# Order of loads and rank items in a fused attention and two-layer kernel, with extra TensorE products at the start

## The reference

```python
a   = softmax(phi, axis=2)                       # phi: 8 x 8 x 576 x 32, over the 32 memory slots
k_m = einsum('bhsm,bhsd->bhmd', a, k)            # 32 x 64 per head
v_m = einsum('bhsm,bhsd->bhmd', a, v)
attn = softmax(q @ k_m^T / 8, axis=-1)           # 576 x 32 per head
x = (attn @ v_m), heads side by side             # 4608 x 512
h = x @ w_in;  g = where(h > 0, h, exp(min(h, 0)) - 1);  x = g @ w_out        # 512 -> 2048 -> 512
h = x @ w2_in; g = h * clip(h + 3, 0, 6) / 6;            out = g @ w2_out     # 512 -> 2048 -> 512
```

## Time and profile before

| what | value |
|---|---|
| median of three runs | 1538.38 us (1538.25 to 1538.83) |
| profiled execution, its time | 1538.7 us |
| profiled execution, its span | 1537.0 us |
| PE busy | 1499.0 us, 98% |
| DVE, ACT, POOL busy | 660.1, 623.5, 126.1 us |
| mean granted TensorE clock | 0.992 |
| L270 of the up passes (pT_hi, w_lo), x512 | 153.2 us busy, 14.4 us idle before |

### The profile page before, as it was taken

The page is one execution under the profiler, slowest core; times in us unless marked ns, Lnnn a source line. Parts: engine busy times, 40 slices in busy tenths (PEclk is TensorE's granted clock), DMA queues, the critical chain, the costliest instruction groups (busy, mean ns, idle before and its releaser), DMA issues.

```text
span 1537.0 us, 24660 instructions
## 1 busy us (share of the span) xinstructions
PE 1499.0 (98%) x9680; PEld 1306.2 (85%) x9680; DVE 660.1 (43%) x1180; ACT 623.5 (41%) x1284; POOL 126.1 (8%) x85
## 2 busy tenths in 40 slices
PE   3999999999999999999999999999999999999999
PEld 2889989889998989999988888888888888888887
DVE  4456565555656556555432222323232222323222
ACT  2655555555555555566632222222222222222222
POOL 0310000000000000003730000101010010101000
PEclk8899999999999999999999999999999999999999
DMA  9732233333222333141300101010100101010000
GB/s 230 190 63 51 52 62 55 71 71 66 59 53 47 61 70 71 28 155 47 126 1 3 53 0 55 1 55 0 55 0 0 55 0 55 0 55 0 27 0 27
DMA packets 155060, 79.49 MB, mean 52 GB/s; under 512 B 117072, under 2 KB 137552, under 8 KB 154960
## 3 DMA queue, kind: packets, MB, share of 16 engines
q1 hardware_dynamic: 151792, 76.67, 19.8%
q10 hardware_dynamic: 3168, 1.47, 0.5%
HBM read 59.24 MB, written 18.87 MB: 51 GB/s over the span
## 4 chain that ended last, share of the span: by engine, by line
PE 90%; ACT 3%; DVE 3%; SPq 2%; issue 1%; DMA 0%; POOL 0%; ACTq 0%; DVEq 0%
PE ps L270 30%; PE ps L272 29%; PE ps L271 29%; PE ps L329 1%; PE ps L297 1%; DVE g L675 1%; ACT g L513 1%; ACT g L511 1%; SPq L829 1%; PE ps L318 1%; SPq L842 1%; DVE w_lo L664 1%; DVE g_lo L682 1%; ACT g_hi L519 0%; DMA w_in_raw<-in_moe_w_in 0%
## 5 line engine op out<-in xcount | busy, mean ns | idle before, releaser
L270 PE MATMUL ps<-g_hi,w_out_lo 128*128 128x288 f32 x1024 | 313.6, 306 | 1.4 <-POOL w_out_lo L761 0.8
L271 PE MATMUL ps<-g_lo,w_out_hi 128*128 128x288 f32 x1024 | 301.9, 295 | 0.0
L272 PE MATMUL ps<-g_hi,w_out_hi 128*128 128x288 f32 x1024 | 301.8, 295 | 0.0
L688 DVE SCALAR_TENSOR_TENSOR g<-g,ps 128x512 f32<-128x512 f32 x144 | 99.1, 688 | 450.6 <-ACT g L525 450.6
L525 ACT ACTIVATE g<-ps,one_half 128x512 f32<-128x512 f32 x144 | 99.3, 690 | 465.7 <-PE ps L272 465.7
L270 PEld LDWEIGHTS ps<-g_hi,w_out_lo 128*128 128x128 f32 x1024 | 192.4, 188 | 38.8 <-issue 24.3
L270 PE MATMUL ps<-x_hi,w_in_lo 128*128 128x512 f32 x576 | 224.1, 389 | 0.0
L271 PE MATMUL ps<-x_lo,w_in_hi 128*128 128x512 f32 x576 | 224.1, 389 | 0.0
L272 PE MATMUL ps<-x_hi,w_in_hi 128*128 128x512 f32 x576 | 224.1, 389 | 0.0
L271 PE MATMUL ps<-w_out_lo,g_hi 128*128 128x512 f32 x576 | 224.1, 389 | 0.0
L270 PE MATMUL ps<-w_out_hi,g_lo 128*128 128x512 f32 x576 | 224.1, 389 | 0.0
(11 more groups left out here) (90 smaller groups left out, 1774.9 us busy)
## 6 DMA issues: line engine op xcount, KB each, us to landing
q_sq<-in_q SPq DMA_DIRECT2D x256, 36.0 KB, 1.9
layer_out<-y_sb SPq DMA_DIRECT2D x16, 576.0 KB, 3.0
x_raw<-layer_out SPq DMA_DIRECT2D x9, 1024.0 KB, 6.9
kv<-in_k SPq DMA_DIRECT2D x15, 576.0 KB, 5.5
kv<-in_v SPq DMA_DIRECT2D x60, 144.0 KB, 5.5
w_in_raw<-in_moe_w_in SPq DMA_DIRECT2D x8, 1024.0 KB, 8.1
w_out_raw<-in_moe_w_out SPq DMA_DIRECT2D x8, 1024.0 KB, 5.9
out<-out_sb SPq DMA_DIRECT2D x8, 1024.0 KB, 5.2
```

The lines of the kernel that those rows point to most:

```text
L270: nc.tensor.matmul(dst, a_lo, b_hi, start=first, stop=False)
L271: nc.tensor.matmul(dst, a_hi, b_lo, start=False, stop=False)
L272: return nc.tensor.matmul(dst, a_hi, b_hi, start=False, stop=last)
L688: nc.vector.scalar_tensor_tensor(g, g, 1.0, hid(f, BLOCK), ALU.min, ALU.mult).then_inc(turn_over, 1)
```

## The change

Three edits. (1) `items_in`: in unit 0 items 2 and 3 move from f=1 and 4 to f=4 and 8; in odd units item 0 moves from f=9 to f=8. (2) SP: `w_in` quarter 2 is issued ahead of k and v of unit 2, and `w_out` quarter 1 ahead of `w_in` quarter 3 and of q of unit 1. (3) PE: a new function `in_use` multiplies the identity with itself (float32, 128x128 by 128 columns) into a bank that nobody reads: 16 times before the first sums of keys and values, 3 times after the scores of unit 0, 4 times after item 0 and 6 times after item 1.

```diff
         def items_in(u, parity):
             if isinstance(u, int) and u == 0:
-                return {1: 2, 4: 3}
+                return {4: 2, 8: 3}
...
-            return {9: 0, 12: 1, 15: 2} if parity else {1: 3}
+            return {8: 0, 12: 1, 15: 2} if parity else {1: 3}
...
+            def in_use(times, bank):
+
+                for _ in range(times):
+                    nc.tensor.matmul(ps[:, bank, 0:P], ident[:, :], ident[:, :], start=True, stop=True)
+
...
-                elif f == 9:
+                elif f == 8:
                     pe.wait_ge(kvT_made, g + 1)
...
                 elif f == 15:
                     pe.wait_ge(w1_lo_made, 2 * (2 * u + 4))
                 elif f == 1:
-                    pe.wait_ge(w1_lo_made, 2 * item_index(u, 0, items_in(u, 0)[f]))
+                    pe.wait_ge(w1_lo_made, 2 * (2 * u + 3))
...
             pe.wait_ge(ident_ready, 1)
             for stage in MEMORY:
+                if stage == S_KV:
+                    in_use(16, HID)
                 memory(0, stage, A)
                 memory(1, stage, B_)
             scores_inputs(0, 2, 0)
             scores(0)
+            in_use(3, ACC)
             item_inputs(0, 0, 2)
             item(0, HID, 0)
+            in_use(4, ACC)
             item_inputs(1, 1, 2)
             item(1, ACC + 2, 0)
+            in_use(6, ACC)
             half(0, 0)
...
             def load_memory(b, gi):
 
                 sp.dma_start(A.rows[0:ROWS], group(phi_d, b, gi)).then_inc(A.phi_loaded, 16)
+                load_keys_values(b, gi)
+
+            def load_keys_values(b, gi):
                 sp.dma_start(A.k[0:ROWS], group(k_d, b, gi)).then_inc(A.kv_loaded, 16)
...
             sp.wait_ge(kv_done, 1)
-            load_memory(1, 0)
+            sp.dma_start(A.rows[0:ROWS], phi_d[:, 1, 0]).then_inc(A.phi_loaded, 16)
             load_in(2, 0, w1_in_loaded[2])
+            load_keys_values(1, 0)
+            load_out(1, 0)
             load_in(3, 0, w1_in_loaded[3])
             sp.wait_ge(qT_made, 2)
             load_q(0, 1)
-            for i in range(1, 4):
+            for i in range(2, 4):
                 load_out(i, 0)
```

## The result

The changed kernel takes 1527.55 us in the median of four runs (1526.64 to 1528.40), the kernel before beside it 1538.32 (1538.16 to 1538.83). The ratio is 0.9926 with a 95% interval of 0.9910 to 0.9942: 10.8 us faster, where 8.2 were forecast (1530.1). A later job gave it 1527.60 (five runs). The profiled execution has a span of 1525.1 us, 11.9 less than before; its time is 1528.4, of which 3.3 lie outside the span, against 1.7 before.

A forecast was written before the change was run, and what follows sets the result against it. PE, busy 98% of the span, was taken as the bound, with some 38 us idle to win. Terms -4.3 - 6.9 + 1.1 + 0.5 + 1.3 = -8.3 gave 1530.1 us, range 1526.5 to 1534.5.

The forecast's parts named there:

- Steady units: Step 10 of odd units: item 0 at step 8 removes seven waits of 0.61 us, 4.3 us off, bounds 0 and 4.5.
- Unit 0, loads and chain: Unit 0: the 5.3 us wait for w_in goes, the ACT, DVE and POOL chain then sets the pace; 6.9 us earlier.
- The milestone: Start of the sums of keys and values in step 5 of unit 0: 49.2 us instead of 56.10.
- Item 3 at step 8: Unit 0: item 3 still comes after the sums of keys and values, its products adding 1.1 us.
- The added products: Before and in early unit 0: the first 16 cost and gain 0; the four hold item 1 back by 1.4 us.
- the 0.5: Start of unit 0: the added products make up1(0) start at 32.9 instead of 32.4, +0.5 us, bounds -0.5 and +2.7.
- The clock: Unit 0, gaps between 34 and 38 us: one more step at the lower clock, +1.3 us, between 0 and 3.3.
- rival A: Unit 0: clock stays up from 30, perhaps already at the scores; no 1.3, -0.5 instead of +0.5; 1527.8 us, chance 0.20.
- B: Unit 0: added products don't raise the clock, only take time; +2.7 and +3.3 replace 0.5 and 1.3; 1534.3 us, chance 0.14.
- C: Odd units: item 0 at step 8 meets a new wait of the same size in step 9 or 12; 1534.4 us, chance 0.11.
- D: Unit 0: a full queue holds SP's issues of q, DVE waits in step 8; +14.5, 1544.6 us, chance 0.05.

The follow-up runs named there:

- the part alone: The kernel before with only item 0 of odd units moved from step 9 to step 8: 1532.65 us, ratio 0.9958.
- the kernel with the early splits: The changed kernel with ACT splitting slices 0 and 1 of w_out ahead of step 0 of unit 0: 1525.53 us; without the 16 products 1525.13.
- the run that asked for it early: The changed kernel with items 2 and 3 of unit 0 back at steps 1 and 4, new order of loads kept: 1529.83 us.

## Why the prediction was right, and its terms

**Steady units.** Right in mechanism: seven waits gone, nothing late in their place, 1.75 us of slack in unit 3 where 1.9 were forecast. The size was off: 7 x 0.61 = 4.3 was forecast, and the part alone measures 6.0. The step that failed is "7 x 0.61", which took the bracket for the cost: by start-to-start distances it is 7 x 0.87 = 6.1. In the change the stretch saves 5.6. The loop's two jumps back take 0.2 of the missing 0.5 (waits of 1.69 and 1.05, before 1.08 and 1.46); the rest is not traced. These two waits are also what the prediction's count left out: of the nine of the earlier trace rows, it placed one ahead of unit 0, and its series of seven has only six under this name.

**Unit 0, loads and chain.** The milestone was put at 49.2 and came at 48.57. Each stop on the way was within 0.2: L685 of step 0 ended at 34.86 (forecast 34.75), the next L685 began at 37.44 (37.5), L521 of step 2 at 38.77 (38.95). Item 3 at step 8 cost 1.1 as forecast: the gain over before drops by 1.11 between two down1 steps there. k and v, q and w_out were hidden as said. Quarter 2 of w_in was put at 35 and landed at 35.6 in the run that asked for it early.

**The added products.** Cost and gain of the 16 were put at 0; they cost 1.3 us by the run without them, though only 0.4, within the scatter, in the kernel with the early splits. The four did hold item 1 back, to 29.36 (1.4 was forecast, it is 0.9), and the six end at 31.97 and hold nothing; up1(0) starts 9.54 us behind the scores as before (9.52). So the 0.5 was 0.

**The clock.** The 1.3 for one more fall in unit 0 did not come: rival A's main condition held, the clock at 1.00 from 30 on. That its 1527.8 is nearly the measured time is partly luck: its term for the steady units was too small by 1.3, and its 0.5 for an upper level at the scores did not come (they took 1.21 us). The rule of the Trainium skill, "TensorE: Matmul & The Clock Gate", section "Why this matters for your kernels", gave 0 for this term, and the windows agree: 1.00 through gaps of up to 1 us between 34 and 44. That short gaps always keep it is not so: in before it fell at about 23 behind waits of 0.49 and 1.41 parted by work, as the prediction says. What I overlooked weighs more: without any products the clock is back by 38 by itself, once the wait for w_in no longer cuts the passes of steps 0 to 2. The products' 13 small ones are worth 0.75 us in unit 0, not the 3.3 that I had as the most.

**The sum.** Forecast -8.3: -4.3 steady and -4.0 up to unit 1. Measured in the span: -5.6 steady, -6.2 in the segment and -0.1 ahead of it, -11.9 in all; in the medians -10.8. B and C did not happen. D did not either: q of unit 1 was issued in 12.76 us, from 39.67 to 52.4, though 2.9 later than I had put its end, and it was still in time.

## What to carry to other kernels

The bracket before a matmul pass showed less than the wait cost here: count from start to start and take off the usual distance (0.87 against 0.61). Before warming PE with idle products, look whether the real passes behind will run without a gap once the true wait (here a load in the wrong place of the queue) is gone; then they can raise the clock themselves, as they did here by 36 to 38 us. The late products brought 0.75 us in unit 0, and all 29 together nothing. Move a load and its user together: either alone left 2.2 to 5.7 us of the gain behind. And when a stage moves forward, look at every load that it uses, not only at the one that was waited for: w_out quarter 1 became the next stop.

## What the runs showed of the hardware

- With 16 float32 products running on PE from 9 to 14 us, SP's issue of 16 small transfers took 12.8 to 13.5 us in six profiles; without them 11.8 to 12.0 in eight. Why is open.
- With five products added ahead of a loop, PE had waits of 1.73 and 1.66 us, released by nothing that the profile shows, behind the loop's two jumps back, with the loop's own code unchanged; the stretch took 4.0 us more than without them. That the length of the code ahead is the cause is inferred from this one case.
- The recorded clock of 1.00 stood over stretches that ran at half rate: in the first 9 us always (L288's pair in 0.74 us, 0.38 at 48 us), and in one profile up to about 37 us, with the item at 1.96 us against 1.09. Durations decide.
- The granted clock stayed at 1.00 through PE waits of 1.84 and 2.55 us in one profile, fell in a wait of 7.62 us in another, and in that of before fell at about 23 behind waits of 0.49 and 1.41 us.
- A DVE subtraction of 128x288 with both inputs in SBUF took 1.28 us beside a POOL subtraction and 0.44 without. L685, which reads one of its inputs from PSUM, took 0.45 beside one (at 41.95 in the changed kernel).
